# Moving the streamed operands of an attention and feed-forward kernel to other places modulo 512 bytes

## What is computed

```python
def reference(q, k, v, proj, w_val, conv_w, w_out, mu_k, mu_r, w_k, w_v, w_r):
    # attention with a mask: a query sees only keys whose 6 sign bits (x @ proj > 0) are its own
    mask = bucket(q @ proj)[..., :, None] == bucket(k @ proj)[..., None, :]
    scores = where(mask, q @ k.T / sqrt(64), -1e9)
    x = softmax(scores) @ v                            # (2, 8 heads, 768, 64) -> (2, 768, 512)
    gate = sigmoid(causal_conv5(x, conv_w))
    x = (gate * (x @ w_val)) @ w_out                   # 512 -> 512 -> 512
    prev = shift(x, 1)
    xk = mu_k * x + (1 - mu_k) * prev
    xr = mu_r * x + (1 - mu_r) * prev
    k = maximum(xk @ w_k, 0)                           # 512 -> 1024
    return sigmoid(xr @ w_r) * ((k * k) @ w_v)         # 1024 -> 512
```

## The kernel before, in words

| stream and its weights | weights at | stream at before | distance before |
|---|---|---|---|
| x, y, xk, xr (high and low) on `w1_hi`, `w1_lo` | 128 | 416 | 288 |
| h_hi, h_lo on `w2_hi`, `w2_lo` | 416 | 416 | 0 |
| k1, k2 on q1, q2, all three sets | 416 | 416 | 0 |
| `ident` on `probs` (transposes, L681) | 160 | 416 | 256 |

## Time and profile before

### The profile page before, as it was taken

The page is one execution under the profiler, slowest core; times in us unless marked ns, Lnnn a source line. Parts: engine busy times, 40 slices in busy tenths (PEclk is TensorE's granted clock), DMA queues, the critical chain, the costliest instruction groups (busy, mean ns, idle before and its releaser), DMA issues.

```text
span 486.8 us, 9484 instructions
## 1 busy us (share of the span) xinstructions
PE 475.1 (98%) x3541; PEld 403.4 (83%) x3541; DVE 350.5 (72%) x611; ACT 279.2 (57%) x597; POOL 257.9 (53%) x254
## 2 busy tenths in 40 slices
PE   8899999999999999999999999999999999999997
PEld 6766677676676676667679998999999999999997
DVE  4887897988889888887687986884786588226211
ACT  4977878887787887876645533451442353244230
POOL 5795547284463746451267546464456458246140
PEclk9999999999999999999999999999999999999999
DMA  6210310304031030200220001001000000000101
GB/s 229 66 55 18 116 37 25 114 16 136 16 97 58 1 135 18 72 18 18 88 86 1 3 1 43 1 1 45 2 2 32 12 2 19 27 1 12 34 1 43
DMA packets 10557, 20.69 MB, mean 42 GB/s; under 512 B 1680, under 2 KB 6928, under 8 KB 10512
## 3 DMA queue, kind: packets, MB, share of 16 engines
q1 hardware_dynamic: 10224, 19.94, 12.5%
q10 hardware_dynamic: 288, 0.15, 0.1%
HBM read 16.94 MB, written 3.15 MB: 41 GB/s over the span
## 4 chain that ended last, share of the span: by engine, by line
PE 78%; DVE 11%; issue 4%; ACT 3%; DMA 2%; POOL 1%; SPq 0%; DVEq 0%; ACTq 0%; POOLq 0%
PE ps L717 28%; PE ps L705 14%; PE ps L725 12%; PE ps L681 10%; PE ps L670 10%; DVE gate L898 2%; DMA raw_k<-kT 2%; ACT probs L482 2%; PE ps L691 2%; DVE tmp_a L971 1%; DVE negmax L855 1%; DVE pt L862 1%; DVE tmp_b L969 1%; PE ps L653 1%; DVE x L888 1%
## 5 line engine op out<-in xcount | busy, mean ns | idle before, releaser
L855 DVE TENSOR_REDUCE negmax<-ps 128x1 f32<-128x768 f32 x96 | 91.7, 956 | 23.7 <-PE ps L670 22.6
L670 PE MATMUL ps<-k,q 128*128 128x384 f32 x384 | 91.9, 361 | 3.1 <-ACT probs L482 2.5
L482 ACT ACTIVATE probs<-ps,negmax 128x768 f32<-128x768 f32 x96 | 86.6, 902 | 9.8 <-DVE negmax L855 9.4
L681 PE MATMUL ps<-ident,probs 128*128 128x128 f32 x576 | 82.4, 275 | 1.9 <-ACT pt L490 0.7
L681 PEld LDWEIGHTS ps<-ident,probs 128*128 128x128 f32 x576 | 66.7, 140 | 12.8 <-DVE pt L862 4.7
L670 PEld LDWEIGHTS ps<-k,q 128*128 128x128 f32 x384 | 62.7, 189 | 14.8 <-ACT probs L482 10.2
L705 PE MATMUL ps<-pt,vals 128*64 128x384 f32 x384 | 68.8, 494 | 0.0
L436 POOL TENSOR_TENSOR h_lo<-tmp_b,h_hi 128x256 fp32r<-128x256 f32 x48 | 38.7, 812 | 45.9 <-ACT h_hi L584 45.9
L490 ACT ACTIVATE pt<-ps 128x384 f32<-128x384 f32 x96 | 47.0, 489 | 19.7 <-PE ps L681 15.9
L862 DVE COPY pt<-ps 128x384 f32<-128x384 f32 x96 | 52.2, 543 | 3.7 <-PE ps L681 3.7
L725 PE MATMUL ps<-h_hi,w_hi 128*128 128x256 f32 x192 | 54.3, 283 | 0.0
(11 more groups left out here) (87 smaller groups left out, 1124.8 us busy)
## 6 DMA issues: line engine op xcount, KB each, us to landing
w_raw<-w SPq DMA_DIRECT2D x8, 640.0 KB, 6.9
raw_q<-qT SPq DMA_DIRECT2D x8, 384.0 KB, 5.8
raw_k<-kT SPq DMA_DIRECT2D x8, 384.0 KB, 3.5
vals<-v SPq DMA_DIRECT2D x16, 192.0 KB, 2.3
out<-w_raw SPq DMA_DIRECT2D x24, 128.0 KB, 1.7
w_raw<-w SPq DMA_DIRECT2D x4, 512.0 KB, 3.2
codes_b<-codes ACTq DMA_DIRECT2D x1, 128.0 KB, 4.1
proj_bd<-proj ACTq DMA_DIRECT2D x1, 16.0 KB, 3.3
```

Of the source, the lines that this page charges most:

```text
L482: act.activation(probs[par][:, :], score[par], ACT.Exp, bias=negmax[:, t:t + 1], accum_out=sums[:, t, 0:1]).then_inc(exp_done, 1)
L670: last = pe.matmul(ps[:, 2 * par + half, 0:HALF], qq[h][:, q], kk[h][:, half * HALF:(half + 1) * HALF], start=first, stop=not first)
L681: last = pe.transpose(tbank[u][:, k * P:(k + 1) * P], probs[g % 2][:, kt * P:(kt + 1) * P], ident[:, :])
L855: dve.tensor_reduce(negmax[:, t:t + 1], score[g % 2], AX.XY, ALU.max, negate=True).then_inc(max_done, 1)
```

## The change

The program's instructions and their order are the same on every engine; only addresses differ. Empty tensors (`apart_...`) are put in between. In the attention, the keys of two of three sets move, by 160 bytes in set 1 and by 288 in set 2, and a second filler brings the queries back to their old place modulo 512. In the feed-forward half each of the ten streamed tensors gets a distance of its own; the weights `w2` move as well, from 416 to 32, `w1` does not.

```diff
@@ -51,6 +51,8 @@
 
 SETS = 3
 
+APART_SETS = (0, 160, 288)
+
 
 def wait(eng, sem, count):
     if count > 0:
@@ -106,6 +108,10 @@
     with ctx:
         def sb(name, shape, dt=F32, stack=ctx):
             return stack.enter_context(nc.sbuf_tensor(name, shape, dt))
+
+        def apart(name, size, stack=ctx):
+
+            return sb(f"apart_{name}", [P, size // 4], F32, stack)
 
         def sem(name):
             return ctx.enter_context(nc.semaphore(name))
@@ -128,9 +134,18 @@
         for n in range(SETS):
             s = (NHEADS + n) % SETS
             q1[s] = sb(f"q1_{s}", [P, SEQ], F32R, att)
+
+            if APART_SETS[s]:
+                apart(f"k1_{s}", APART_SETS[s], att)
             k1[s] = sb(f"k1_{s}", [P, SEQ], F32R, att)
+            if APART_SETS[s]:
+                apart(f"q2_{s}", 512 - APART_SETS[s], att)
             q2[s] = sb(f"q2_{s}", [P, SEQ], F32R, att)
+            if APART_SETS[s]:
+                apart(f"k2_{s}", APART_SETS[s], att)
             k2[s] = sb(f"k2_{s}", [P, SEQ], F32R, att)
+            if APART_SETS[s]:
+                apart(f"end_{s}", 512 - APART_SETS[s], att)
         pt0 = sb("pt0", [P, KT, SEQ], F32, att)
         vals = [sb(f"vals{h}", [P, KT, DH], F32, att) for h in range(2)]
         bits = sb("bits", [P, HALF], BF16, att)
@@ -149,8 +164,15 @@
         pt = [pt0, pt1]
         att.close()
 
-        x_hi, x_lo = sb("x_hi", [P, DT, GQ], F32R), sb("x_lo", [P, DT, GQ], F32R)
-        y_hi, y_lo = sb("y_hi", [P, DT, GQ], F32R), sb("y_lo", [P, DT, GQ], F32R)
+
+        apart("x_hi", 32)
+        x_hi = sb("x_hi", [P, DT, GQ], F32R)
+        apart("x_lo", 32)
+        x_lo = sb("x_lo", [P, DT, GQ], F32R)
+        apart("y_hi", 32)
+        y_hi = sb("y_hi", [P, DT, GQ], F32R)
+        apart("y_lo", 32)
+        y_lo = sb("y_lo", [P, DT, GQ], F32R)
         tmp_a = sb("tmp_a", [P, 2, GQ])
         tmp_b = sb("tmp_b", [P, 2, GQ])
         w2_raw = sb("w2_raw", [P, 2, W2_PIECE])
@@ -160,9 +182,17 @@
         for n in range(2):
             w2_hi.append(sb(f"w2_hi{n}", [P, W2 // 2], F32R))
             w2_lo.append(sb(f"w2_lo{n}", [P, W2 // 2], F32R))
-        h_hi, h_lo = sb("h_hi", [P, FT, GQ], F32R), sb("h_lo", [P, FT, GQ], F32R)
-        xk_hi, xk_lo = sb("xk_hi", [P, DT, GQ], F32R), sb("xk_lo", [P, DT, GQ], F32R)
-        xr_hi, xr_lo = sb("xr_hi", [P, DT, GQ], F32R), sb("xr_lo", [P, DT, GQ], F32R)
+        apart("h_hi", 160)
+        h_hi = sb("h_hi", [P, FT, GQ], F32R)
+        apart("h_lo", 32)
+        h_lo = sb("h_lo", [P, FT, GQ], F32R)
+        xk_hi = sb("xk_hi", [P, DT, GQ], F32R)
+        apart("xk_lo", 32)
+        xk_lo = sb("xk_lo", [P, DT, GQ], F32R)
+        apart("xr_hi", 128)
+        xr_hi = sb("xr_hi", [P, DT, GQ], F32R)
+        apart("xr_lo", 192)
+        xr_lo = sb("xr_lo", [P, DT, GQ], F32R)
         recept = sb("recept", [P, DT, GQ])
         z = sb("z", [P, DT, 1 + GQ])
```

## The result

The changed kernel takes 489.44 us (median of 22 runs, 489.06 to 490.69) against 488.57 us before (22 runs): a ratio of 1.0018 with a 95% interval of 1.0012 to 1.0025. It is slower by 0.9 us, where 1.5 us less were forecast. The time lies inside the whole range of 482.5 to 491.0 us, which had been widened for rival A, but above the forecast's own range of 485.0 to 488.3 and on the other side of "before". Two executions of this study are left out of all times as disturbed: one of the kernel before (2,613 us) and one of e5 (518.9 us), which is the one that was profiled.

What follows compares the result with a forecast made beforehand. PE's matmul pace was taken to bound the last stage. From the profiled 488.57 us, L725's 1.5 us less and zero for the other terms gave 487.1, against the median 487.0 us; own range 485.0 to 488.3, whole range 482.5 to 491.0.

Steps and rivals of the forecast that it cites:

- rival A: Feed-forward: 288 was a good place; L717's eight new distances at L725's pace cost 3.5 us more, 492.1 us; chance 0.22.
- The bound: Last stage, from 297.5 us: PE is busy without a gap, so time is the number of matmuls times their pace.
- Term 1: L725 (h), distance 0 to 160 and 192: 480 matmuls at 116.7 instead of 119.9 ns, 1.5 us less.
- Term 2: L717, distance 288 to eight others, 1,104 matmuls: no change; bounds 8.5 us less to 3.5 us more.
- Term 3: Attention scores, ten of 16 heads, 240 matmuls: zero; bounds 3.6 us less to 1.2 us more.
- Term 4: Other engines using the moved tensors: no cost, with slack of over 80 us each from 297.5 us on.
- The signs: Wrong if L717's pieces leave 28.0 us by over 0.5 or scores' groups 0.70 by over 0.03; paces within 2 ns of 116.7.
- Rival B: Matmul series: pace does not depend on distance, the 3.2 ns come from something else; 488.5 us; chance 0.20.
- Rival C: L717 and L725: most places beat both, paces 112.8 and 114.5 ns, 6.9 us less, 481.6 us; chance 0.12.

Runs made afterwards that it cites:

- e5: Kernel before with only the change's key moves (sets at 0, 160, 288), feed-forward half as before: 488.49 us against 488.55, ratio 1.0001.
- e6: Kernel before with only h_hi and h_lo moved, to 160 and 192: 487.84 us against 488.55, ratio 0.9985.
- e7: Kernel before with only the eight streams on w1 moved to the change's places, h at 0, keys as before: 490.33 us against 488.55, ratio 1.0038.
- e1 to e3: Kernel before with high and low part of each stream at equal distances, a different set per run, keys as before: 488.75, 488.74 and 488.76 us beside 488.86.
- e8: Kernel before with all ten streams at distance 192, keys as before: 486.84 us, ratio 0.9968.
- e10: Kernel before with xr and h at 192, x, y and xk at 288 as before: 485.31 us, ratio 0.9934.
- e11: Kernel before with all streams at 192 except xk at 128, and keys at 64, 96 and 448: 487.83 us (one run).
- e1: Kernel before with both parts of x at 0, y 64, xk 128, xr 192, h 288, keys as before: 488.75 us (one run) beside 488.86.
- e8 to e10: Kernel before with streams moved to 192: all ten (486.84 us), only h (487.70 us), or h and xr (485.31 us).
- e12: Kernel before with streams at x 176, y 208, xk 200, xr 184, h 196 and all keys at 192: 491.49 us (one run) beside 488.48.

## Why the prediction was wrong

**The bound** was right. PE still fills the last stage without a gap, no wait came or went, and the pieces of the chain add up to 0.9 us more (1.9 less 1.0).

**Term 1, L725**, was right in its sign and half again too large: 0.20 us per stretch, 1.0 us in all, instead of 1.5; 117.8 ns instead of 116.7. The time of e6 alone says 0.7 us. Why h at 160 and 192 runs at 117.8 is open.

**Term 2, L717, is the step that failed**: "I take no change ... as long as only 0 is special". It was 1.9 us more in the chain and 1.8 us in e7. Zero is not special: 96 is as dear as 0 and so is 256, and of the twelve equal distances tried beside 288 only 32, 192 and 448 are as cheap as 288 or cheaper. A single value from one place was taken for the typical value of all others, while the term multiplies it by 1,104. Its upper bound, 119.9 ns and 3.5 us, held.

**Term 3, the scores**, zero, held: the groups keep their 0.70 us, e5 is within 0.1% of before, and the steps show 0.2 us. **Term 4** held too: no other engine entered the chain of the last stage.

**The signs** were partly too coarse. The prediction was to be wrong if L717's pieces left 28.0 us by more than 0.5; they left it by 0.4, which over 4.6 chunks is 1.9 us, more than the whole forecast gain. The sign that did speak was the other one: paces within 2 ns of 116.7, where xk ran at 119.0. That the stated range holds the time is owed to rival A, for which it was widened, and not to the mechanism of the forecast.

**Rival A** was what happened, with the chance of 0.22: 288 was a good place. It was sized at 492.1 us with all of L717 at 119.9 ns and L725 unchanged; in fact L717's mean rose by 1.7 ns, just beyond the stated point of decision of 1.4 ns, and L725's gain took 1.0 us back. Its reason, a slope with nearness to 0, was wrong: 32 is cheap and 256 is dear. **Rival B**, no dependence, is refuted by e1 to e3: the instructions are the same and only addresses differ. The rule that the prediction quotes from the Trainium skill ("TensorE: Matmul & The Clock Gate", "Step-by-step: what each phase is for") says that loading the next weights takes no read bandwidth from the running matmul. The step from there to "the distance cannot matter" is refuted by these paces; whether the read ports are the place where the time is lost, no run here shows. **Rival C** was right that paces far below both known ones exist, 113.3 ns at 192 and 448, and wrong that most places are so: of the twelve, ten are not, and the change has only h_lo and xr_lo at those two.

What could have been seen beforehand: the two known points differed by 3.2 ns in 117, and the term with 2.3 times the matmuls started from the cheaper one. With nothing known of eight new places, the mean of the two points, not the lower one, is the fairer guess for them: 118.3 ns, 1.6 x 1,104 = 1.8 us more for L717 and 0.8 us less for L725. That this comes so near the measured 1.9 and 1.0 is partly luck: the mean of the twelve equal distances tried later is 117.6 ns, and the change happened to hold dearer ones.

## What to carry to other kernels

Where matmuls of four-byte operands follow each other without a gap and each loads new weights, the start of the streamed tensor counted from its weights moves the pace, here between 113.3 and 121.7 ns for 256 columns. Read the pace from pieces of the chain, not from recorded durations, and measure a sweep of distances in one kernel, a distance per tensor, before choosing any. If a change moves several series off a place, the one with the most matmuls deserves the care, and its present place is one draw that may be a lucky one. Since one distance can have two paces, measure the kernel as a whole before a new place is kept: e8 put all ten streams at the cheapest distance and was slower than e10, which put only xr and h there.

## What the runs showed of the hardware that was not expected

- The pace repeats with 256 bytes, in all five pairs tried: 119.6 and 119.8 ns at 0 and 256, 117.9 and 117.7 at 64 and 320, 118.6 and 118.8 at 128 and 384, 113.3 and 113.3 at 192 and 448, 116.7 and 116.7 at 32 and 288.
- One distance can hold two steady paces: 113.3 and 117.8 ns at 192, 118.7 and 120.0 at 128 (e11), 116.9 and 117.8 at 288 (h in e1). In e8 to e10 a stretch of 96 matmuls at 192 keeps one of the two but for its first few, and a kernel can alternate between them from chunk to chunk (e11). What selects it is open.
- All five streams that began off a multiple of 32 bytes from their weights ran at 119.4 to 121.7 ns (e12).
- The distance matters more than the address: with the weights `w1` at 128 modulo 512 and `w2` elsewhere, 0 gave 119.6 and 119.9 ns (`w2` at 416; 120.0 with `w2` at 32, e7), 64 gave 117.9 and 117.8 (`w2` at 224), and 192 gave 113.3 and 113.5 (`w2` at 416, and at 320 in e8). At 160 the two differed by 1.2 ns (`w2` at 448), at 288 by 1.1 (`w2` at 192). For the streams on `w1` alone, distance and address were never told apart.
